# Recurrent attention into two MLPs: the first block's tiles become two-batch chunks of 64 tokens, and four row tiles of the first MLP are done in two halves of the columns, one half between the attention tiles

## The reference, cut to what matters

```python
def _attn_ref(q, k, v, alpha):           # (4, 8, 768, 48) each
    for t in range(S):
        state = alpha[:, :, t, :, None] * state + np.einsum('bhd,bhe->bhde', k[:, :, t], v[:, :, t])
        y[:, :, t] = np.einsum('bhd,bhde->bhe', q[:, :, t], state)
...
x = np.ascontiguousarray(attn_out.transpose(0, 2, 1, 3)).reshape(B * S, H * D)   # (3072, 384)
h = x @ w_in;  g = h * np.clip(h + 3.0, 0.0, 6.0) / 6.0;  x = g @ w_out           # w_in (384, 2048), w_out (2048, 384)
h = x @ w_in2; r = np.maximum(h, 0.0); g = r * r;         x = g @ w_out2
```

## Time and profile before

| | us |
|---|---|
| median of 3 executions | 860.66 (860.63 to 860.75) |
| the profiled execution | 859.13 |
| its span, first to last instruction | 857.4 |
| TensorE busy in the span | 849.5 |

### The profile page before, as it was taken

How to read it: one execution, slowest core, us unless ns; L and a number is a source line. 1 busy time by engine, 2 the same in 40 slices (tenths; PEclk the granted TensorE clock), 3 DMA queues, 4 the chain that set the end, 5 groups by cost and what they waited for, 6 DMA issues and landing times.

```text
span 857.4 us, 15319 instructions
## 1 busy us (share of the span) xinstructions
PE 849.5 (99%) x6312; PEld 703.7 (82%) x6312; DVE 331.1 (39%) x466; ACT 327.9 (38%) x586; POOL 316.6 (37%) x248
## 2 busy tenths in 40 slices
PE   8999999999999999999999999999999999999998
PEld 7888888888888888888888888888888888888886
DVE  8977545564455555421333311212211211211111
ACT  4754433343434333333445423333323333323332
POOL 2855443344433443433333333333333333333332
PEclk9999999999999999999999999999999999999999
DMA  9743233332233332200323001000000000100101
GB/s 351 296 108 96 40 95 87 90 78 72 71 81 100 86 80 75 61 16 5 111 74 111 0 1 38 1 0 26 12 1 8 29 1 0 37 1 1 37 0 39
DMA packets 67496, 51.84 MB, mean 60 GB/s; under 512 B 50785, under 2 KB 57185, under 8 KB 67425
## 3 DMA queue, kind: packets, MB, share of 16 engines
q1 hardware_dynamic: 67424, 50.84, 19.4%
HBM read 40.60 MB, written 8.26 MB: 57 GB/s over the span
## 4 chain that ended last, share of the span: by engine, by line
PE 97%; DMA 1%; SPq 0%; ACT 0%; issue 0%; ACTq 0%
PE h_ps L1046 46%; PE o_ps L1059 46%; PE att_all L939 1%; PE att_all L923 1%; DMA w_in_raw<-w_in 1%; PE att_all L990 1%; PE att_all L1014 1%; SPq L400 0%; PE h_ps L976 0%; ACT k_tok L561 0%; PE att_all L901 0%; PE att_all L976 0%; SPq L406 0%; SPq L402 0%; ACT squares L549 0%
## 5 line engine op out<-in xcount | busy, mean ns | idle before, releaser
L522 POOL TENSOR_TENSOR g_parts<-h_act,g_parts 128x512 fp32r<-128x512 f32 x192 | 257.8, 1343 | 518.9 <-ACT g_parts L603 518.8
L1059 PE MATMUL o_ps<-g_parts,w_out_hi 128*128 128x512 f32 x1152 | 327.0, 389 | 0.0
L1046 PE MATMUL h_ps<-x_parts,w_in_hi 128*128 128x512 f32 x1152 | 295.3, 392 | 0.0
L1059 PEld LDWEIGHTS o_ps<-g_parts,w_out_hi 128*128 128x128 f32 x1152 | 216.1, 188 | 45.0 <-POOL g_parts L522 0.2
L1046 PEld LDWEIGHTS h_ps<-x_parts,w_in_hi 128*128 128x128 f32 x1152 | 214.4, 188 | 45.3
L603 ACT ACTIVATE g_parts<-h_act 128x512 fp32r<-128x512 f32 x192 | 121.3, 632 | 271.4 <-PE o_ps L1059 241.5
L787 DVE SCALAR_TENSOR_TENSOR h_act<-h_ps,h_gate 128x512 f32<-128x512 f32 x96 | 66.3, 691 | 290.5 <-ACT h_gate L598 290.5
L1059 PE MATMUL o_ps<-g_parts,w_out_lo 128*128 128x512 f32 x576 | 165.6, 389 | 0.0
L1046 PE MATMUL h_ps<-x_parts,w_in_lo 128*128 128x512 f32 x576 | 161.7, 389 | 0.0
L1046 PEld LDWEIGHTS h_ps<-x_parts,w_in_lo 128*128 128x128 f32 x576 | 108.1, 188 | 22.6
L1059 PEld LDWEIGHTS o_ps<-g_parts,w_out_lo 128*128 128x128 f32 x576 | 108.1, 188 | 22.5
(11 more groups left out here) (114 smaller groups left out, 375.8 us busy)
## 6 DMA issues: line engine op xcount, KB each, us to landing
inputs<-att_in SPq DMA_DIRECT2D x18, 772.0 KB, 4.5
w_in_raw<-w_in SPq DMA_DIRECT2D x8, 768.0 KB, 7.8
w_out_raw<-w_out SPq DMA_DIRECT2D x8, 768.0 KB, 9.1
result<-inputs SPq DMA_DIRECT2D x18, 256.0 KB, 2.4
inputs<-v_in SPq DMA_DIRECT2D x20, 192.0 KB, 2.8
k_tok<-turned_keys SPq DMA_DIRECT2D x18, 192.0 KB, 2.9
x_mid<-att_in SPq DMA_DIRECT2D x4, 772.0 KB, 8.9
turned_keys<-x_mid SPq DMA_DIRECT2D x36, 64.0 KB, 2.3
```

The lines of the kernel that those rows point to most:

```text
L522: nc.gpsimd.tensor_tensor(g_parts[:, g % 2, 1, :], h_act[:, g % 2, :], g_parts[:, g % 2, 0, :].bitcast(F32), ALU.subtract).then_inc(g_lo, 1)
L1046: last = nc.tensor.matmul(h_ps[g % 2][:, :], w[:, m, cols], x_parts[:, n % 2, part, m, :], start=m == 0 and i == 0, stop=m == KT - 1 and i ...
L1059: return nc.tensor.matmul(o_ps[m][:, :], w[:, f, m * P:(m + 1) * P], g_parts[:, g % 2, part, :], start=f == 0 and w is w_out_hi and part = ...
```

## The change

**Tiles.** All 24 tiles are now 64 tokens of two batches. Tiles 0 and 1 open all four batches and have no state before them (`STATELESS = 2`). Tiles 2 and 3, of the first block too, now read a state (`first_visit`, `carry_on_padded`), wait for `decay_state` and for a new copy `tail_state`, and have their keys turned and sent through DRAM, as tiles from 4 on had before. Tiles 0 and 1 still turn their keys on TensorE. Keys of all four first tiles are scaled on VectorE; before, GpSimd did tiles 1 and 2.

**Half units.** Row tiles f = 0 to 3 of the first MLP's first block are each done in two units of 256 columns. Units g = 0 to 3 (`OPENING = 4`) take the first half, the tokens of tiles 0 and 1, and stand between the tiles; units 4 to 7 take the other half, in steps 0 to 3 of the loop. Everything from step 4 on is of full width. The first visit of the loop moves from step 4 to step 5 (`ATTEND_AT`), and two sums for the state (`add_up_first(2)` and `add_up_first(3)`) now stand in the loop.

**Loads.** The first weight groups come in two pieces, so that the first row tile can start early. Loads of tiles and values and the key traffic of tiles 2 and 3 are interleaved in SyncE's list. Weight group 2 is split before the loop, its low part on GpSimd.

```diff
-ATTEND_AT = (4, 7, 10, 13)
+ATTEND_AT = (5, 8, 11, 13)
-FIRST_SCORE_AT = (3,)
+FIRST_SCORE_AT = (4,)
+STATELESS = 2
+PADDED = BATCH
+OPENING = 4
+LAST_PADDED_SUM_AT = 2
-WARM_UP = (14, 8, 3, 2)
+WARM_UP = (14, 12)
-W1_AT = {2: 1, 3: 3, 4: 4, 5: 6, 6: 7, 7: 10}
+W1_AT = {3: 3, 4: 4, 5: 6, 6: 7, 7: 10}
+def of_unit(g):
+    if g < OPENING:
+        return 0, g, slice(0, BLK // 2)
+    n, f = divmod(g - OPENING, FT)
+    return n, f, slice(BLK // 2 if n == 0 and f < OPENING else 0, BLK)
...
             def store_turned(t):
-                sp.wait_ge(blocks_turned, t - BATCH + 1)
-                past(sp, keys_loaded, 16 * (t - BATCH))
+                sp.wait_ge(blocks_turned, t - STATELESS + 1)
+                past(sp, keys_loaded, 16 * (t - STATELESS))
...
             def turn_blocks(t):
                 dve.wait_ge(k_scaled, t + 1)
-                past(dve, turned_stored, 16 * BLOCKS * (t - BATCH))
+                past(dve, turned_stored, 16 * BLOCKS * (t - STATELESS))
...
         @block.scalar
...
-            copy_keys(0)
             check_from_end(0)
             check_to_token(0)
-            x_high(0)
-            first_state(0)
-            split_w(0)
+            split_first_w(0)
+            split_other_w(0)
+            copy_keys(0)
...
+            high(2)
+            gate(3)
+            high(3)
+            x_high(2)
+            split_w(2)
+            x_high(3)
...
         @block.vector
...
             make_decays(1)
+            scale_keys(1)
+            scale_queries(1)
             mask(0)
-            scale_queries(1)
-            make_decays(2)
             mask(1)
+            x_low(0)
+            x_low(1)
+            make_from_end(2)
+            activate(0)
+            make_to_token(2)
+            scale_keys(2)
+            activate(1)
             scale_queries(2)
+            update_state(0)
+            decay_state(2)
+            make_from_end(3)
+            activate(2)
+            mask(2)
+            make_to_token(3)
+            scale_keys(3)
+            activate(3)
+            scale_queries(3)
+            x_low(2)
+            update_state(1)
+            decay_state(3)
+            mask(3)
+            turn_blocks(2)
+            x_low(3)
+            turn_blocks(3)
             make_from_end(BATCH)
...
         @block.tensor
...
+            attend_alone(0)
+            attend_alone(1)
+            hidden(0)
+            add_up_first(0)
+            hidden(1)
+            hidden(2)
+            project(0)
+            score_alone(2)
+            hidden(3)
+            project(1)
+            first_visit(2)
+            project(2)
+            score_alone(3)
+            project(3)
+            first_visit(3)
+            for step in range(2 * STEPS + LAG):
+                g = OPENING + step
...
+                if step == LAST_PADDED_SUM_AT:
+                    add_up_first(PADDED - 2)
```

More of the change, by code:

```diff
@@ L39 @@
 SEGMENTS = 2 * PAIRS
[L41 removed]
+ALPHA_W = SEGMENTS * PART_REV
 KQ_W = 2 * PAIRS * TILE
@@ L584, in first_state @@
[L584 to L589 removed]
+                for parity in range(2):
+                    nc.scalar.activation(k_tok[:, :, HD * parity:HD * (parity + 1)], keys_by_token(t)[:, :, half_rows(parity)],
+                                         ACT.Copy).then_inc(k_back_copied, 1)
@@ L886, in warm_up, with score @@
             def warm_up(i):
[L887 to L891 removed]
+                for n in range(WARM_UP[i]):
+                    place, width = WARM_PLACES[n if i == 0 and n < len(WARM_PLACES) else -1]
+                    nc.tensor.matmul(banks[:, place:place + width], ident[:, :], ident[:, 0:width], start=True, stop=True)
+            def score(t, clears):
                 pe.wait_ge(k_scaled, t + 1)
                 pe.wait_ge(q_scaled, t + 1)
[L894 to L916 removed]
                 for j in range(PAIRS):
@@ L921, in score_later, with score_alone @@
                             rows = half_rows(parity)
-                            place = SCORE_COLS[parity] + j * PART
-                            last = nc.tensor.matmul(att_all[cols, place:place + PART], keys(t)[rows, j, cols],
-                                                    queries(t)[rows, j, cols], start=parity == 0 or not with_output(t),
+                            place = score_cols(t)[parity] + j * PART
+                            last = nc.tensor.matmul(banks[cols, place:place + PART], keys(t)[rows, j, cols],
+                                                    queries(t)[rows, j, cols], start=parity == 0 or clears,
                                                     stop=True, skip_group_check=True)
                 last.then_inc(scored, 1)
+            def score_alone(t):
+                pe.wait_ge(y_made, t if t > STATELESS else 1)
+                pe.wait_ge(x_hi, x_pieces(t - 1))
+                pe.wait_ge(x_lo, x_pieces(t - 1))
+                pe.wait_ge(state_made, t - 1)
+                score(t, True)
+            def score_later(t):
+                pe.wait_ge(attended, t - STATELESS)
+                score(t, False)
             def carry_on(t, crossed):
@@ L970, in attend_first @@
-                pe.wait_ge(masked, 2 * (t + 1))
-                for m in range(KT):
-                    if t == BATCH - 1 and m == KT - 1:
-                        pe.wait_ge(x_lo, 1)
-                    for kind, j in enumerate((m, TAIL)):
-                        for half in range(2):
-                            last = nc.tensor.matmul(first_y(t, m)[HALF * half:HALF * (half + 1), :],
-                                                    first_values(t)[:, kind, m, half, :], masked_of(t)[:, side_of(j, half), j, :],
-                                                    start=kind == 0, stop=kind == 1)
-                    if t == BATCH - 1 and m < KT - 1:
-                        last.then_inc(last_y_made, 1)
@@ L981, in attend_first @@
-                last.then_inc(y_made, 1)
+                for m in range(KT):
+                    for kind, j in enumerate((m, TAIL)):
+                        for side in range(2):
+                            for b in range(2):
+                                tokens = slice(PART * b, PART * (b + 1))
+                                place = output_cols(t)[b] + m * PART
+                                last = nc.tensor.matmul(banks[HALF * side:HALF * (side + 1), place:place + PART],
+                                                        first_values(t)[tokens, kind, m, side, :],
+                                                        masked_part(t)[tokens, side_of(j, side), j, :],
+                                                        start=m == 0 and kind == 0, stop=True, skip_group_check=True)
```

698 lines of the change are left out of this document (349 added, 349 removed).

## The result

| | before | after |
|---|---|---|
| median of the runs, us | 860.66 (860.63 to 861.11) | 885.15 (883.85 to 886.64) |
| ratio, 95% interval | | 1.0281, 1.0270 to 1.0292 |
| the profiled execution, us | 859.13 | 884.74 |
| span, us | 857.4 | 882.9 |

The change makes the kernel 24.5 us slower. The forecast was 872.8, 12.1 us slower, with a range of 869 to 877 (864 to 878 with its rivals). The sign was right, the size was half of what was measured.

A forecast was written before the change was run, and what follows sets the result against it. TensorE bounds the kernel (busy 849.5 of 857.4 us) after an opening set by VectorE. With tile 4's visit at 59.9 instead of 43.7, 857.4 + 59.9 - 43.7 - 4.1 = 869.5 span, median 872.8, range 869 to 877 (864 to 878 with rivals).

The forecast's parts named there:

- Break-even at 33.5 for `hidden(4)`: End of opening: with 823.9 us left and no later wait, the change breaks even at 33.5; `hidden(4)` expected about 33.8.
- The second count by idle times: Cross-check of the slowdown: later start 7.5, minus 8.16, plus 1.5, idle 11.3 and 0.6 for `x_lo(3)`, makes 12.7 us.
- A half product costs 0.12 us: Later half units in the loop: 72 products of 256 columns at 0.12 us, 8.64 in place of 16.32 us.
- Rival E: Later half units: a half product costs as much as a full one, 0.227 us, 16.3 rather than 8.6; chance 0.02.
- First half unit at 15.0: Opening: TensorE starts its first half unit at 15.0 us, after attention and x parts of tiles 0 and 1.
- GpSimd's contention, 0.8 us: Opening: GpSimd's weight splits slow VectorE's list by 0.8 us, bounds 0 and 4, so `turn_blocks(2)` ends at 32.2.
- The stores, the keys, tile 5, `activate(7)`, the mask: Loop up to tile 4's visit: transposed keys through DRAM cause TensorE idle of 3.0, 1.0, 4.3 and 3.0 us; visit at 59.9.
- Rival D, the clock: Idle ahead of tile 4's visit: clock falls to 1.2 GHz, costing 4.1 us more there, 877 us; chance 0.15.
- After the visit: From tile 4's visit to the end: 809.6 us, loads ahead again, row tiles without a gap at 2.04 us.
- Rival A: Loop loads: not that late, tile 5 arrives before 45, only the first two waits remain, about 865.5 us; chance 0.14.
- Rival B: Opening: VectorE's list is shorter, `turn_blocks(2)` ends at 28 or before, `hidden(4)` at 29 to 30, 858 us; chance 0.10.
- Rival C: Whole kernel: no change, every key transfer hidden, span of 857.7 us, measured time 861 us; chance 0.06.

The follow-up runs named there:

- the best version: As run 11, with the low parts of the first two weight groups also moved from GpSimd to VectorE, all products computed: 869.68 us, ratio 1.0100.
- run 2: Changed kernel with 4 instead of 12 warm-up products in the second series: 881.89 us, ratio 1.0242.
- run 9: Changed kernel with SyncE waiting for mask(1) before issuing the second weight group and everything behind it: 883.16 us, ratio 1.0242.
- Run 1: Changed kernel without GpSimd's weight splits in the opening; ScalarE writes zeros for those low parts, left out of the products: 877.32 us, ratio 1.0186.
- run 4: Changed kernel with `turn_blocks(3)` moved from ahead of the loop into it, behind `activate(5)`: 884.33 us, ratio 1.0279.
- run 7: Changed kernel with sixteen zero products before each of `hidden(6)`, `hidden(9)` and the wait for tile 4's visit: 885.33 us, ratio 1.0285.
- run 12: Changed kernel with the zeros of Run 1 for GpSimd's low parts and the held loads of run 9 together: 876.50 us, ratio 1.0185.
- run 3: Changed kernel with the loads of tile 5 and its values moved right behind tile 4's load: 879.10 us, ratio 1.0207.
- run 5: Changed kernel with `turn_blocks(2)` moved behind `scale_queries(2)` and `turn_blocks(3)` into its old place: 875.35 us, ratio 1.0165.
- run 8: Changed kernel with fewer warm-ups, tile 5 loaded early, tile 2's keys transposed early and weight group 2 split behind `x_high(3)`: 874.63 us, ratio 1.0157.
- run 11: Changed kernel with fewer warm-ups, held loads, early transpose, group 2's low part on VectorE, tile 5 loaded in idle queue, group 3 split earlier: 872.01 us.

## Why the prediction was right in sign and wrong in size

- **Break-even at 33.5 for `hidden(4)`**: it started at 43.73, and in the best version at 38.36. From there to the end the prediction had 823.9 us without waits. The best version takes 869.2 - 38.36 = 830.8; of the 6.9 more, 3.35 are the two waits shown, and about 2, by my estimate, the lower clock behind waits. Some 1.5 stay unaccounted for. Right in the main. (The second count by idle times has a slip: halves and sum make 0.5 + 0.5 = 1.0 by the prediction's own terms, not 1.5.)
- **A half product costs 0.12 us**: right. In the changed kernel three start at 57.25 and the next unit at 57.61. The rule of the Trainium skill on weight loads (TensorE: Matmul & The Clock Gate, "The mechanism" and "LDWEIGHTS (loading the stationary operand)") would have 0.214, the estimate that the prediction worked out from it, and doesn't hold here either. Rival E is out.
- **First half unit at 15.0**: 18.04 measured. This step failed: it took for granted that a product starts when its operands are there, and had no term for anything else. The instructions weren't there (runs 2 and 9). Together with `x_low(1)` being 0.4 later this is 3.4 of the 9.5 us by which `turn_blocks(2)` was late.
- **GpSimd's contention, 0.8 us**: this is the step that failed most. Measured on the six instructions that it hit in the opening (L749, L754, L762, both L767, a scan): 0.8 + 0.2 + 1.8 + 0.4 + 3.1 + 0.4 = 6.6 us more than their time alone, 5.8 above the term, and above its bound of 4. Run 1 shows it without GpSimd's splits. I had read 1.04 and 2.96 as two samples of a slowdown; they are two samples of a wait for the end of whatever GpSimd is at, and its splits here take 3.1 and 3.6. With 3.4 and 5.8 the error of 9.5 is accounted for within 0.3 in this trace. That it comes so close is partly luck: VectorE also waits 0.8 more at `x_low(2)` than in runs 4 and 7, and with both causes taken away (run 12) the transpose ends at 34.18 and not at 32.2. By run time, GpSimd's splits are worth 7.8 us (run 1) and the late instructions 2.0 (run 9) of the 12.4 by which the forecast was short.
- **The stores, the keys, tile 5, `activate(7)`, the mask**: from the end of `turn_blocks(2)` to the visit 27.7 us were foreseen, and it took 28.3. Runs 3, 4 and 5 bear out the chain: loading tile 5 early or turning the keys early takes 6 and 10 us off, taking away one wait in the middle of it takes off nothing.
- **Rival D, the clock**: it fell in idle as described there. Its price at the visit was 1.1 us (run 7), not 4.1: the clock was back within the visit. Elsewhere in the changed kernel the idle behind it covered most of it. That isn't so in every run: in runs 3, 4, 5, 7, 8 and 9 the visit of tile 3 stood at the lower clock, and 4.4 to 4.7 us passed from the end of `mask(3)` to `hidden(4)` where the changed kernel's trace has 3.1. So in those traces up to 1.6 us that VectorE was early were lost again.
- **After the visit** 809.6 us were foreseen and 813.0 measured: 1.3 for the slower visit and 1.5 for a wait for values at 111.94 that I hadn't foreseen; some 0.6 stay open. Of the 1.3, 1.1 are the clock's and 0.2 are `add_up_first(3)`, which I had cost at nothing (2.11 at full clock in run 7, 1.93 before). That the wait at 111.94 comes of the visits at steps 11 and 13 standing closer now was not tested.
- **Rivals A, B and C** are out: tile 5 landed at 60.9, and `turn_blocks(2)` ended at 41.7.

## What to carry to other kernels

When work moves into an opening stage, price it by what the engines do to each other there: lay GpSimd's instructions beside VectorE's in time, and add for each overlap the rest of the GpSimd instruction, not a share. This holds for the copies, scans and two-input instructions of the next section. Where GpSimd's next instruction follows at once, it can be that one too: the scan of 2.96 us in the earlier trace rows ended only after two of them, the second of which ended at 35.63. Put whatever starts a round trip through DRAM as early in its engine's list as its operands allow: run 5 won 9.8 us, more than taking away all of GpSimd's splits did (7.8), although it saved no work. And test a wait by removing it: where a chain of arrivals stands behind it (run 4), its time is not to be had.

## What the runs showed of the hardware that was not expected

**VectorE stands until GpSimd's instruction ends.** A 112x96 copy took 3.25 to 3.29 us in the seven traces where it stood beside the 128x1536 split, and 0.21 without it. All six instructions that were held in the changed kernel's opening follow one sum: they end at the end of GpSimd's instruction plus their own time alone, less 0.12 to 0.15 us. Instructions that read PSUM weren't held: `update_state` took 0.54 and a mask 0.69 beside a split. Nor was a transpose, which has one input: 1.09 in run 5 beside a split. The Trainium skill (SBUF — State Buffer, "Who interferes with whom") says that VectorE's instructions with two inputs in SBUF, and copies in the modes that use both of its port pairs, contend with GpSimd for a shared pair, and that whoever holds it keeps it for a whole instruction; the traces agree in which instructions were held, and in how long, by the ends 40.06 and 39.99.

**TensorE can run out of instructions.** In the runs with a full data queue at the start TensorE stopped behind record 220 in every one (1.4 to 3.8 us), in two more behind 470 or 472 (2.1 and 3.2), in three behind 596 (1.6 to 4.0), and went on each time 1.3 to 1.6 us after the end of one 16 KB packet of the instruction queue. The distance 470 - 220 is 250 products, each with a weight load, and 596 - 470 is 126, half of that. The small products of the tiles use up instructions fastest: 96 in 1.63 us, where a row tile has nine in 2.04. The Trainium skill (Runtime: NRT & Kernel Launch, "Instruction fetch mechanics") has instructions come in blocks of 16 KiB, 256 each, by a DMA queue of the sequencer's own, "mostly hidden". Packet size and distances agree, the distances being about two blocks and one. By an estimate from the page's 256 the 6630 products of the changed kernel and as many weight loads are 52 blocks, and the queue q8 has 53 such packets there; that this queue is TensorE's is inferred from that. Hidden it is not, where many small products meet saturated loads (run 9), and perhaps not without them (run 11).

**Splits cost GpSimd twice what they cost VectorE.** The low part of 128x1152 took 2.62 to 3.09 us there and 1.35 on VectorE. In the opening VectorE was better off doing the work itself than waiting for it: with 3.8 us of splits in its list it was done with `mask(3)` 3.0 us sooner than in run 11.
